# Attention with the products with the values in one piece per group, placed behind the fourth block's transposes

## What is computed

```python
# q, k, v: (2, 8, 768, 64); proj: (64, 6)
mask   = q_bucket[:, :, :, None] == k_bucket[:, :, None, :]   # buckets: signs of q @ proj, k @ proj
scores = where(mask, q @ k.T / sqrt(64), -1e9)
attn   = exp(scores - max(scores)); attn /= attn.sum(-1) + 1e-9
x      = attn @ v                                             # -> (1536, 512), input of both expert layers
```

## Time and profile before

| | before |
|---|---|
| median of 3 runs | 642.27 us (640.92 to 644.3) |
| span of the profiled execution | 638.8 us |
| TensorE busy | 620.4 us, 97% of the span |
| VectorE busy | 360.6 us, 56% |
| ScalarE busy | 295.1 us, 46% |
| L353 (the products with the values), 360 instructions | 68.0 us |
| L338 (transposes of the probabilities), 576 | 78.8 us |
| chain of work that ended last | TensorE 87% of the span |

### The profile page before, as it was taken

One profiled execution on the slowest core, in us unless ns is written; L12 is line 12 of the kernel. 1 busy time (PEld: TensorE's weight loads), 2 busy tenths in 40 slices (PEclk: granted clock), 3 DMA queues, 4 the chain that ended last, 5 costly groups with the idle time before them and its releaser, 6 DMA issues.

```text
span 638.8 us, 11468 instructions
## 1 busy us (share of the span) xinstructions
PE 620.4 (97%) x4384; PEld 484.4 (76%) x4384; DVE 360.6 (56%) x1132; ACT 295.1 (46%) x525; POOL 146.8 (23%) x152
## 2 busy tenths in 40 slices
PE   6999999999999999888999999999999999999997
PEld 3777776777677766367898989898999877777773
DVE  6876777677777776886868778786522220000000
ACT  5867777777776767542525343452212111111111
POOL 5340303031222911210100101010333123333201
PEclk9999999999999999989999999999999999999999
DMA  8947936455464100371634435373798769999970
GB/s 191 235 91 160 216 81 155 108 125 125 109 194 95 47 10 1 113 274 42 249 124 166 157 133 179 135 249 102 271 345 313 268 223 330 353 341 353 335 271 20
DMA packets 73394, 116.38 MB, mean 182 GB/s; under 512 B 33800, under 2 KB 37162, under 8 KB 73059
## 3 DMA queue, kind: packets, MB, share of 16 engines
q1 hardware_dynamic: 68738, 106.75, 54.6%
q0 software_dynamic: 4016, 8.80, 4.0%
q10 hardware_dynamic: 576, 0.01, 0.0%
HBM read 87.76 MB, written 12.23 MB: 157 GB/s over the span
## 4 chain that ended last, share of the span: by engine, by line
PE 87%; issue 6%; DVE 3%; DMA 1%; ACT 1%; POOL 1%; SPq 0%; POOLq 0%; DVEq 0%
PE psB L1061 12%; PE psB L1075 12%; PE psB L353 10%; PE psB L338 9%; PE psB L1807 9%; PE psB L1822 9%; PE psA L323 7%; PE psA L325 5%; PE psB L368 2%; PE psA L997 1%; PE psB L281 1%; PE psB L1098 1%; PE psB L292 1%; PE psB L1992 1%; PE psB L1047 1%
## 5 line engine op out<-in xcount | busy, mean ns | idle before, releaser
L474 DVE TENSOR_REDUCE mx<-psA 128x1 f32<-128x768 f32 x96 | 91.8, 956 | 52.0 <-PE psA L325 50.6
L542 ACT ACTIVATE prob<-psA,ebi,esc 128x768 f32<-128x768 f32 x96 | 95.2, 992 | 23.9 <-DVE ebi L419 19.5
L1061 PE MATMUL psB<-xgT,w 128*128 128x192 f32 x512 | 93.3, 335 | 0.4 <-ACT xgT L1161 0.3
L1061 PEld LDWEIGHTS psB<-xgT,w 128*128 128x128 f32 x512 | 84.2, 193 | 7.1 <-issue 3.8
L1075 PE MATMUL psB<-hT,w 128*128 128x192 f32 x512 | 88.2, 329 | 0.0
L1075 PEld LDWEIGHTS psB<-hT,w 128*128 128x128 f32 x512 | 82.7, 190 | 0.3
L338 PE MATMUL psB<-cst,prob 128*128 128x128 f32 x576 | 78.8, 273 | 0.3
L323 PE MATMUL psA<-kH,qT 128*128 128x384 f32 x192 | 74.2, 387 | 2.8 <-ACT kB L581 1.6
L338 PEld LDWEIGHTS psB<-cst,prob 128*128 128x128 f32 x576 | 66.8, 140 | 5.3 <-DVE pT L487 1.9
L353 PE MATMUL psB<-pT,v_in 128*64 128x384 f32 x360 | 68.0, 499 | 0.0
L593 ACT COPY pT<-psB 128x512 f32<-128x512 f32 x96 | 55.9, 582 | 25.4 <-PE psB L338 24.6
(11 more groups left out here) (289 smaller groups left out, 874.6 us busy)
## 6 DMA issues: line engine op xcount, KB each, us to landing
w<-in_moe_w SPq DMA_DIRECT2D x34, 2048.0 KB
kH<-hi SPq DMA_DIRECT2D x30, 192.0 KB
q_in<-in_q SPq DMA_DIRECT2D x16, 192.0 KB, 3.9
k_in<-in_k SPq DMA_DIRECT2D x16, 192.0 KB, 4.3
v_in<-in_v SPq DMA_DIRECT2D x8, 384.0 KB, 3.4
x_scratch<-x_of_batch SPq DMA_DIRECT2D x2, 1536.0 KB, 6.5
x_scratch<-x SPq DMA_DIRECT2D x8, 384.0 KB
qT<-hi SPq DMA_DIRECT2D x15, 192.0 KB
```

What stands on the lines that cost most here:

```text
L474: nc.vector.tensor_reduce(mx[:, u:u + 1], psS[u % 2][:, :, 0:HALF], AX.XY, ALU.max).then_inc(s_dv, 1)
L542: nc.scalar.activation(prob[:, u % 2, :, :], psS[u % 2][:, :, 0:HALF], ACT.Exp, bias=ebi[:, u:u + 1], scale=esc[:, u:u + 1], accum_out=den ...
L1061: ins = nc.tensor.matmul(ps[:, (f % 2) * CAP:(f % 2 + 1) * CAP], w1[:, k % 2, d, f * P:(f + 1) * P], xgT[:, k % 2, d, :], start=d == 0, st ...
```

## The change

PVC becomes one piece of all six key chunks, and the piece stands behind the transposes of the group's fourth block (n = 3, PIECE_AT) only. Nothing in the work of a product changes: the same 12 products a group, in the same order of chunks. The bits' prep (k = 4), which could be taken at any odd n, can now be taken at n = 3 only (at n = 1 in the first group), behind the piece; since the list todo is worked in order, the later preps move too. In the last group the piece stands behind the third block's transposes, and X of the group before at the fifth.

```diff
         if G == NGRP - 1:
 
-            steps.append([("X", G - 2), ("PV", G - 1, 0), ("PV", G - 1, 1), ("PV", G - 1, 2), ("X", G - 1), None][n])
-            if n == per - 1:
-                steps.pop()
+            steps += [[("X", G - 2)], [], [("PV", G - 1, 0)], [], [("X", G - 1)], []][n]
             continue
-        if G and n % 2:
-            steps.append(("PV", G - 1, n // 2))
+        if G and n == PIECE_AT:
+            steps.append(("PV", G - 1, 0))
         if G > 1 and n == 0:
             steps.append(("X", G - 2))
...
-        elif todo and todo[0][2] == 4 and n % 2:
+        elif todo and todo[0][2] == 4 and n == (PIECE_AT if G else 1):
             steps.append(todo.pop(0))
...
-PVC = [[0, 1], [2, 3], [4, 5]]
+PVC = [[0, 1, 2, 3, 4, 5]]
+
+PIECE_AT = 3
```

## The result

| | before | changed |
|---|---|---|
| median | 642.37 us of 6 runs (640.92 to 644.3) | 657.11 us of 6 runs (654.1 to 660.57) |
| span of the profiled execution | 638.8 us | 655.4 us |

The ratio is 1.0235, with a 95% interval of 1.0206 to 1.0264: the changed kernel is slower by 14.7 us at the medians and by 16.6 us between the two profiled executions. The forecast was 657.3 us, in a range of 650 to 667. In a second set of runs on another occasion the ratio was 1.020 (1.0159 to 1.0242).

What follows compares the result with a forecast made beforehand. TensorE bounds steady attention, its product pieces hiding a loop through the other engines. Terms 11.3 + 3.6 - 0.4 - 1.6 + 1.8 = 14.7, say 15 us, added to the 642.27 median give 657.3 us, range 650 to 667.

Steps and rivals of the forecast that it cites:

- The bound: Steady attention: TensorE full, 14.87 us a group; blocks without products run at 1.88 us each through the other engines.
- the loop's pace: Scores, maximum, copy, scale, exponentials, then the scores after next: 3.75 us for two blocks, 1.88 a block.
- The entry, 0.16 and 0.19: Product pieces: 0.16 us to enter, 0.19 to leave; one 4.00 us piece saves 0.70 us of TensorE a group.
- The window: Six blocks between one piece and the next, no products between: 11.35 us, bounds 11.26 and 12.0.
- One sign: Stretch of two steady groups: TensorE's busy share falls to about 90%, 28.3 of 31.5 us.
- The whole: All of attention: 11.3 + 3.6 - 0.4 - 1.6 + 1.8 = 14.7, say 15 us slower.
- the walk: Blocks a to f timed from a piece's end: waits of some 0.7 us at c, 0.3 at e, 0.5 at f.
- VectorE's work behind X: Seven casts after X0 and two reductions after X9, ahead of block d's reduction, no longer hidden: +1.8 us.
- Step 5: Moved preps and the copy to xun cost nothing; placing 12.4 us against 16.1 available, some 4 us of slack.
- A: Rival: TensorE stays the bound in attention and the saved entries are a gain, 631.8 us; chance 0.05.
- B: Rival: a pair's operand placing is late, say 3 us at each of six pairs, 675 us; chance 0.05.
- C: Rival: TensorE's clock drops to half in each of 15 windows, 1.7 us each, 682 us; chance 0.03.

Runs made afterwards that it cites:

- the one-chunk kernels: Changed kernel and kernel before, each with 10 of a group's 12 products left out, only key chunk 0 multiplied: 620.88 and 622.7 us.
- the longer loop: Four extra one-column VectorE operations ahead of each block's scale: kernel before 644.04 us (ratio 1.0051), changed kernel 667.21 us (1.0412).
- the six-piece kernel: Kernel before with six pieces of one key chunk, one behind each block's transposes: 659.69 us, ratio 1.0242.
- the changed kernel with the scale first: Changed kernel with VectorE's scale of block u + 2 put ahead of its copy of block u's transposes: 655.52 us, ratio 1.0225.

## Why the prediction was right

**The bound.** That a block without products behind it runs at the loop's pace is shown three ways: the chain of waits in the windows, the one-chunk kernels, and the longer loop (three times its added length a window, 1.46 us in two groups, where the kernel before takes 0.22).

**The entry, 0.16 and 0.19.** Measured 4.02 us for the piece (4.00 forecast), and 2.39 us for the six additional ways in and out of two groups of the six-piece kernel (2.10 by the forecast's price; that kernel waits for xun, too). Right. The page on tiling (the Trainium skill, TensorEngine Tiling (Array Packing), Key Properties) says that a change of tiling mode drains the engine; the rows agree in sign, and a change that follows it alone loses here.

**The window.** 11.27 us, forecast 11.35. Two groups 31.29, forecast 31.5. One sign was wrong: TensorE's busy share was to fall to about 90%, and it is 96% (30.06 of 31.29). The sign counted work as it adds up in a stream, 28.3 us, and that is what TensorE had to do; the profile's busy time counts a score that waits for its whole 0.44.

**The whole.** The parts in the traces: to the first piece (35.98, before 30.91) +5.1, where +3.6 was forecast (two blocks at 1.88 would be 3.8; the sum has 3.6); 13 periods from 35.98 to 242.14, 206.16 us against 192.93 (30.91 to 223.84), +13.2, forecast 11.3 + 1.8 = 13.1; the last period 13.96 against 14.33, -0.4, forecast -0.4; the end 8.85 against 10.23, -1.4, forecast -1.6. The sum is 16.5 between these two executions, forecast 14.7.

Of the 1.8 missing 1.5 are at the very start, and they are probably not the change: how soon the first q and k land differs from run to run. From 12 to 30 us TensorE waits for DMAs 0.95 us in the changed kernel (0.45 for kH, 0.50 for q_in), 2.2 in the kernel with only the preps moved, and not at all in the kernel before. In the profiled runs of kernels with a piece at n = 1 the first piece began at 30.8 (the one of before), 31.4, 31.5, 32.2, 32.3 and 33.7 us. With the first piece at n = 3 it was 35.3 to 36.4, in six. The middle of the first kind is 31.9, of the second 36.0, 4.1 us apart, near the two blocks.

That the 13 periods came out at 13.1 is luck in part. The steady groups lose 1.55 us in two, 10.1 in 13, and 11.3 was forecast. What comes on top is 3.1, and 1.8 was forecast: the first period is 1.50 us longer than a steady one (the seven casts, 0.80, and 0.60 in which TensorE waits ahead of the first X product, a wait that the changed kernel's profile of the second set doesn't have), the one with the two reductions 0.98, and the one behind it 0.64, where a copy to raw and its transposes (L393) stand in the chain; the walk had nothing for the 0.60 and the 0.64. The two errors cancel.

At the medians the change costs 14.7, and the forecast 15 (14.7 rounded). The second set gave 13.6 and the profiled pair 16.6, so an agreement to the tenth says nothing.

**VectorE's work behind X.** The changed kernel's chain goes through the casts after X0 (47.68 to 48.48, 0.80 us) and through both reductions after X9 (0.98), as the prediction had it. The second:

```profile
189.18 0.47 DVE x_of_batch L510
189.65 0.77 DVE M L886
...
190.64 0.87 DVE mx L474
```

**The moved preps.** Step 5 called them free. The placing is in time: from the last issue to the scores it is 8.3 us, where the prediction's numbers make it 16.1 - 9.9 = 6.2. But the bits' product, which the sum carried along with its 0.39 us a group, needn't have cost that: inside the window it is nearly free (11.47 against 11.27 + 0.78). I had the number right and the reason incomplete: with the bits at an odd n as before, the one piece costs 12.6 us at the medians (654.73 against 642.17), and 2 to 4 of the 15 come from keeping the bits behind the piece. The kernel with only the preps moved gives them some 2 us (0 to 4.6), not measured well enough to say more.

**The rivals.** A (TensorE stays the bound) needs scores that don't wait; they waited 34 times. B needs a placing that is late; none was. C needs a lower clock; it was 1.00 in all windows shown and from 30 to 265 us, with scores that wait about three times a group. The Trainium skill (TensorE: Matmul & The Clock Gate, Part 4 on the PE-mode transpose) says that transposes don't count as busy for the clock, which had made this rival one to be feared; no run here shows such an effect, with transposes for nearly half of TensorE's work between pieces.

## What to carry to other kernels

When the bound engine's work is rearranged and not reduced, ask what latency its pieces had covered: write down the loop through the other engines (here 3.75 us for two blocks) and compare it with what the bound engine has between two passes of it, block by block and not on the mean. A stretch of the kernel where the cover is missing anyway, as the start was here, measures the new state before it exists. Work that is mostly free in one place (0.58 of the bits' 0.78 us in a window that waits) costs its full length in another (behind the piece), so filler belongs where the waits are.

## What I had not expected of the hardware

The size of what a piece costs to enter and leave is very even: 4, 8, 12 and 24 matmuls of 384 columns took 0.80, 1.44, 2.09 and 4.02 us, always 0.16 to 0.18 above 0.16 each, and the score behind any of them 0.37 or 0.38 instead of 0.18.

And 0.18, 0.37 and 0.44 are one and the same score instruction. It is 0.42 to 0.45 us long in each case; what differs is how much of it lies beside the work ahead of it. In the timeline of the changed kernel, behind transposes without and with a wait:

```profile
136.47 0.82 PE L338 MATMUL psB<-cst,prob 128*128 128x128 f32 x6
137.04 0.42 PE L323 MATMUL psA<-kH,qT 128*128 128x384 f32 x1
...
137.84 0.82 PE L338 MATMUL psB<-cst,prob 128*128 128x128 f32 x6
139.18 0.44 PE L323 MATMUL psA<-kH,qT 128*128 128x384 f32 x1 [0.52 <-ACT prob L542]
```

The first starts 0.25 us before the transposes end (137.29), the second 0.52 behind their end (138.66). So being late costs the wait and the lost overlap of some 0.25 us besides, which the engine's idle time doesn't show. There are cases in between: in the changed kernel with the scale first a score starts at 137.09, only 0.09 us before its transposes end, and the chain counts 0.35 for it.
